# Six digits instead of seven in the threshold search of an expert routing

## What is computed

```python
def _moe_ref(x, w_gate, w1, w2):
    cap = N // E                                   # 2304 // 8 = 288
    order = np.argsort(-(x @ w_gate).flatten())
    for idx in order:                              # best pairs of row and expert first
        tok, e = (int(idx) // E, int(idx) % E)
        if assigned[tok] >= 0 or counts[e] >= cap:
            continue
        assigned[tok] = e; counts[e] += 1
    for e in range(E):
        out[mask] = np.maximum(x[mask] @ w1[e], 0.0) @ w2[e]
def _moe2_ref(x, w_in, w_out, alpha):
    h = x @ w_in
    return (np.maximum(h, 0.0) + alpha * np.minimum(h, 0.0)) @ w_out
```

## Time and profile before

| | us |
|---|---|
| three runs | 1071.69, 1072.57, 1073.44 |
| median | 1072.57 |
| span of the profiled execution | 1067.7 |
| device time of the profiled execution | not listed; its span is 4.9 below the median of the runs |
| PE, DVE, ACT, POOL busy | 926.5, 702.5, 370.7, 357.0 |

### The profile page before, as it was taken

The page is one execution under the profiler, slowest core; times in us unless marked ns, Lnnn a source line. Parts: engine busy times, 40 slices in busy tenths (PEclk is TensorE's granted clock), DMA queues, the critical chain, the costliest instruction groups (busy, mean ns, idle before and its releaser), DMA issues.

```text
span 1067.7 us, 23789 instructions
## 1 busy us (share of the span) xinstructions
PE 926.5 (87%) x8288; PEld 871.3 (82%) x8288; DVE 702.5 (66%) x1860; ACT 370.7 (35%) x1093; POOL 357.0 (33%) x332
## 2 busy tenths in 40 slices
PE   4788898991159999998999899899989999999996
PEld 3677787881148998998899799889979998999995
DVE  6787978758855775675577557656765775675342
ACT  5666676654322114212311321241133124214311
POOL 4463635337545025303601430270144026105401
PEclk9999999995559999999999999999999999999999
DMA  7726363117531212021211202120230212023000
GB/s 156 166 62 148 78 141 79 31 38 196 160 105 44 59 55 71 24 80 47 80 53 54 79 24 80 45 75 23 75 95 24 80 44 68 16 80 102 23 1 22
DMA packets 122571, 76.99 MB, mean 72 GB/s; under 512 B 64328, under 2 KB 105288, under 8 KB 122440
## 3 DMA queue, kind: packets, MB, share of 16 engines
q1 hardware_dynamic: 119368, 65.83, 23.1%
q0 software_dynamic: 3072, 9.44, 3.0%
HBM read 65.81 MB, written 9.44 MB: 70 GB/s over the span
## 4 chain that ended last, share of the span: by engine, by line
PE 58%; DVE 15%; issue 12%; ACT 7%; POOL 6%; DMA 1%; SPq 0%; DVEq 0%; POOLq 0%; ACTq 0%
PE bank L927 15%; PE bank L929 14%; PE bank L928 14%; ACT prob L573 3%; POOL w1s L1414 3%; PE bank L937 3%; DVE onehot L1143 3%; PE bank L390 2%; POOL turning L1422 2%; DVE place L1141 2%; ACT kT L565 2%; PE bank L326 2%; DVE place L1142 2%; DVE nbias L483 1%; PE bank L405 1%
## 5 line engine op out<-in xcount | busy, mean ns | idle before, releaser
L1382 ACT CAST hid<-act 128x288 fp32r<-128x288 f32 x128 | 55.4, 433 | 361.7 <-DVE act L1239 361.7
L927 PE MATMUL bank<-hid,wout 128*128 128x288 f32 x512 | 155.9, 304 | 5.4 <-DVE hid L1245 5.4
L927 PE MATMUL bank<-xy,win 128*128 128x288 f32 x512 | 155.2, 303 | 2.3 <-DVE xy L1230 2.3
L929 PE MATMUL bank<-hid,wout 128*128 128x288 f32 x512 | 152.5, 298 | 0.0
L928 PE MATMUL bank<-hid,wout 128*128 128x288 f32 x512 | 151.3, 296 | 0.0
L928 PE MATMUL bank<-xy,win 128*128 128x288 f32 x512 | 151.3, 295 | 0.0
L929 PE MATMUL bank<-xy,win 128*128 128x288 f32 x512 | 150.8, 294 | 0.0
L1422 POOL DMA_INDIRECT turning<-x_rows,id_new x24 | 24.2, 1007 | 349.6 <-DVE id_new L1213 344.7
L1237 DVE TENSOR_SCALAR neg<-bank,alph 128x288 f32<-128x288 f32 x128 | 66.2, 517 | 101.0 <-PE bank L929 98.9
L1414 POOL TENSOR_TENSOR w1s<-raw,w1s 128x512 fp32r<-128x512 f32 x64 | 86.5, 1353 | 115.7 <-ACT w1s L1351 115.5
L573 ACT ACTIVATE prob<-bank,nbias 96x102 f32<-96x102 f32 (+1 forms) x256 | 86.7, 346 | 50.2 <-DVE nbias L483 34.2
(11 more groups left out here) (184 smaller groups left out, 2254.2 us busy)
## 6 DMA issues: line engine op xcount, KB each, us to landing
raw<-in_moe_w SPq DMA_DIRECT2D x128, 256.0 KB, 3.4
qn<-in_q SPq DMA_DIRECT2D x48, 96.0 KB, 2.3
kn<-in_k SPq DMA_DIRECT2D x48, 96.0 KB, 2.4
vn<-in_v SPq DMA_DIRECT2D x4, 1152.0 KB
x_rows<-xs SPq DMA_DIRECT2D x24, 192.0 KB, 2.1
raw<-in_moe_w_in SPq DMA_DIRECT2D x16, 256.0 KB, 4.0
raw<-in_moe_w_out SPq DMA_DIRECT2D x16, 256.0 KB, 3.7
vw<-in_v SPq DMA_DIRECT2D x16, 204.0 KB
```

The source lines that it names most:

```text
L927: nc.tensor.matmul(out_ap, a_hi, b_hi, start=start, stop=False)
L929: return nc.tensor.matmul(out_ap, a_hi, b_lo, start=False, stop=stop)
L1382: nc.scalar.copy(hid[:, (FC + j) % 3, 0, :], act[:, j % 2, :]).then_inc(h_hi, 1)
```

## The change

The key is read as digits of 5, 5, 5, 5, 6 and 6 bits. There are six levels; levels 4 and 5 compare with 64 values instead of 32 (1536 elements on DVE, products of 64 columns on PE). The digits get their radix added by two instructions instead of one. `PIECES` falls from 18 to 16. The eight low halves that DVE makes in the first routing stood at pieces 2, 4, ... 16; now they stand at 2, 4, ... 14 and 15.

```diff
+DIGIT_BITS = [5, 5, 5, 5, 6, 6]
...
-    BITS = J.bit_length() - 1
-    SHIFTS = list(range((32 - 1) // BITS * BITS, -1, -BITS))
-    LEVELS = len(SHIFTS)
+    LEVELS = len(DIGIT_BITS)
+    SHIFTS = [sum(DIGIT_BITS[l + 1:]) for l in range(LEVELS)]
+    RADIX = [1 << bits for bits in DIGIT_BITS]
...
-    at_least = onehot[:].rearrange("p t m -> p (t m)")[:, 0:NT * J].rearrange("p (t j) -> p t j", t=NT)
+    flat_onehot = onehot[:].rearrange("p t m -> p (t m)")
+    at_least = [flat_onehot[:, 0:NT * j].rearrange("p (t j) -> p t j", t=NT) for j in RADIX]
...
+            radix = RADIX[i // 2]
             if i % 2 == 0:
                 for t in range(NT):
-                    last = nc.tensor.matmul(pR[0:E, 0:J], choice[:, t, :], at_least[:, t, :],
+                    last = nc.tensor.matmul(pR[0:E, 0:radix], choice[:, t, :], at_least[i // 2][:, t, :],
                                             start=(t == 0), stop=(t == NT - 1))
             else:
-                last = nc.tensor.matmul(pR[0:T, 0:J], f["ones"][0:E, :], enough[:], start=True, stop=True)
+                last = nc.tensor.matmul(pR[0:T, 0:radix], f["ones"][0:E, :], enough[:, 0:radix], start=True, stop=True)
...
             do(v.tensor_copy(digits[:], digits_i[:]))
-            do(v.tensor_scalar(digits[:, 1:, :], digits[:, 1:, :], float(J), None, ALU.add), wait=False)
+            for l in range(1, LEVELS):
+                if RADIX[l] != RADIX[l - 1] or l == 1:
+                    same = [m for m in range(l, LEVELS) if set(RADIX[l:m + 1]) == {RADIX[l]}]
+                    do(v.tensor_scalar(digits[:, l:same[-1] + 1, :], digits[:, l:same[-1] + 1, :], float(RADIX[l]), None,
+                                       ALU.add), wait=False)
...
-                    do(v.tensor_scalar(any_v[:], pR[0:T, 0:J], 0.0, None, ALU.is_gt, ALU.add, accum_out=reach[:]))
-                    do(v.tensor_scalar(here, place[:, (l - 1) % 2, :], reach[:], float(J), ALU.subtract, ALU.mult))
+                    do(v.tensor_scalar(any_v[:, 0:above], pR[0:T, 0:above], 0.0, None, ALU.is_gt, ALU.add, accum_out=reach[:]))
+                    do(v.tensor_scalar(here, place[:, (l - 1) % 2, :], reach[:], float(radix), ALU.subtract, ALU.mult))
...
-    DVE_UNIT = {2 * m + 2: m for m in range(DVE_RES)}
+    DVE_UNIT = {min(2 * m + 2, PIECES - 1): m for m in range(DVE_RES)}
```

More of the change, by code:

```diff
@@ L799, in experts @@
     J = f["digit_at"].shape[1]
-    BITS = J.bit_length() - 1
-    SHIFTS = list(range((32 - 1) // BITS * BITS, -1, -BITS))
-    LEVELS = len(SHIFTS)
+    LEVELS = len(DIGIT_BITS)
+    SHIFTS = [sum(DIGIT_BITS[l + 1:]) for l in range(LEVELS)]
+    RADIX = [1 << bits for bits in DIGIT_BITS]
+    assert sum(DIGIT_BITS) == 32 and max(RADIX) == J
     RAW = 8
@@ L1079, in experts @@
     n_steps = [0]
-    STEPS = 9 + LEVELS + 3 + 3 * (LEVELS - 1) + 4 + 7 + 5 + 4 + 3 + 7 + 5 + 3 + 2
+    STEPS = 9 + LEVELS + 2 + len(set(RADIX[1:])) + 3 * (LEVELS - 1) + 4 + 7 + 5 + 4 + 3 + 7 + 5 + 3 + 2
     def stepper(e, k):
@@ L1116, in dve_prepare @@
             for l, shift in enumerate(SHIFTS):
-                do(v.tensor_scalar(digits_i[:, l, :], key[:], shift, J - 1, ALU.logical_shift_right, ALU.bitwise_and),
+                do(v.tensor_scalar(digits_i[:, l, :], key[:], shift, RADIX[l] - 1, ALU.logical_shift_right, ALU.bitwise_and),
                    wait=l == LEVELS - 1)
@@ L1135, in dve_route @@
             l = i // 2
+            radix, above = RADIX[l], RADIX[l - 1]
             here = place[:, l % 2, :]
@@ L1138, in dve_route @@
                 if l > 0:
-                    do(v.tensor_scalar(any_v[:], pR[0:T, 0:J], 0.0, None, ALU.is_gt, ALU.add, accum_out=reach[:]))
-                    do(v.tensor_scalar(here, place[:, (l - 1) % 2, :], reach[:], float(J), ALU.subtract, ALU.mult))
+                    do(v.tensor_scalar(any_v[:, 0:above], pR[0:T, 0:above], 0.0, None, ALU.is_gt, ALU.add, accum_out=reach[:]))
+                    do(v.tensor_scalar(here, place[:, (l - 1) % 2, :], reach[:], float(radix), ALU.subtract, ALU.mult))
                     do(v.tensor_tensor(here, here, digits[:, l, :], ALU.add))
-                ask(v.tensor_tensor(at_least, bc(here, 2, [T, NT, J]), bc(f["digit_at"][:], 1, [T, NT, J]), ALU.is_ge))
+                each = [T, NT, radix]
+                ask(v.tensor_tensor(at_least[l], bc(here, 2, each), bc(f["digit_at"][:, 0:radix], 1, each), ALU.is_ge))
             else:
-                ask(v.tensor_scalar(enough[:], pR[0:E, 0:J], cap8[:], None, ALU.is_ge))
+                ask(v.tensor_scalar(enough[:, 0:radix], pR[0:E, 0:radix], cap8[:], None, ALU.is_ge))
         elif i == 2 * LEVELS:
-            do(v.tensor_scalar(any_v[:], pR[0:T, 0:J], 0.0, None, ALU.is_gt, ALU.add, accum_out=reach[:]))
+            above = RADIX[LEVELS - 1]
+            do(v.tensor_scalar(any_v[:, 0:above], pR[0:T, 0:above], 0.0, None, ALU.is_gt, ALU.add, accum_out=reach[:]))
             here = place[:, (LEVELS - 1) % 2, :]
@@ L1502, in attention_then_experts @@
     E = w_gate.shape[1]
-    T, J = 96, 32
+    T, J = 96, 1 << max(DIGIT_BITS)
     NT = B * S // T
@@ L1520, in attention_then_experts @@
         fixed = route_consts(nc, lasting, T, NT, E, J)
-        early = early_buffers(lasting, T, NT, E, J, LEVELS=7, JT=NT // E, RAW=8, DM=H * D, FC2=w_in.shape[1] // 128)
+        early = early_buffers(lasting, T, NT, E, J, LEVELS=len(DIGIT_BITS), JT=NT // E, RAW=8, DM=H * D, FC2=w_in.shape[1] // 128)
         psum = [whole.enter_context(nc.psum_tensor(f"bank{i}", [128, 512], F32)) for i in range(8)]
```

## The result

The changed kernel takes **1056.36 us** (median of 4 runs, 1050.43 to 1056.88) against 1072.13 for the kernel before in the same session: a ratio of 0.9834, with a 95% interval of 0.9806 to 0.9863. So it is faster by about 16 us; the forecast was 6.5 (1066.1), and its range ended at 1061.5. The profiled execution took 1056.76 us with a span of 1055.0. It lies near its median, and the one before lies low: the spans differ by 12.7 us and the medians by 15.8, so the traces can account for 12.7 only.

A forecast was written before the change was run, and what follows sets the result against it. PE was taken to bound the looped passes, DVE and POOL the first routing. Passes -5.3 and first routing -1.2 made -6.5 us off the median 1072.57: 1066.1 us, range 1061.5 to 1070.8.

The forecast's parts named there:

- one level less: Looped passes: PE loses one level of small products with the gaps at its edges, -1.1 us a pass, -7.7 in all.
- 64 columns on PE, two levels: Looped passes: 24 products of 64 columns cost PE 0.05 us more a level, +0.7 over fourteen levels.
- level 4 waits for DVE: Looped passes: DVE's wider comparison uses up 0.58 us of slack, so PE waits 0.2 a pass, +1.5 in all.
- level 5 delays `xy`: Looped passes: no slack, so 0.80 us of wider comparison delays the low half the first `third` needs, +5.6 in all.
- the tail wait: End of a pass: PE's 0.78 us wait for unit 14's low half goes as the preparation moves earlier, -5.4 in all.
- The first routing: Head before the looped passes: -3.5 for a level, +1.6 comparisons, +0.6 PE columns, +0.1 additions, together -1.2 us.
- the low half that leaves level 6: First routing: 1.7 us of level 6's 6.33; it moves to a later piece, so not counted as saved.
- the collisions of level 6: First routing: POOL operations that collided with level 6 hit what follows, so 3.5 us saved was taken instead of 4.6.
- 2, "more is won": No wait at level 4, whole contended level gained in the first routing, two fewer collisions: -11.1, 1061.5 us; chance 0.13.
- 1: End of a pass: the wait moves one step earlier instead of going, -1.1 in all, 1071.5 us; chance 0.14.
- 3: Looped passes: one more POOL operation ahead of DVE, 1.27 us a pass, +2.4 in all, 1075.0 us; chance 0.06.
- 4: PE's products of 64 columns cost their columns in full, 0.34 us: +4.0, 1070.1 us; chance 0.07.

The follow-up runs named there:

- the kernel whose `xy` waits for PE: The changed kernel with digits of 5, 5, 6, 5, 5, 6 bits and piece 9 given two places instead of one; 1072.58 us.
- the fastest kernel: The changed kernel with digits 5, 5, 6, 5, 5, 6, pieces 9 and 0 two places long, first running-sum part two places instead of three; 1043.65 us.

## Why the prediction was wrong, point by point

**The failed step: what bounds the kernel.** The prediction took a looped pass to be PE at work "with short waits", and its sum compares two passes by the pieces and their order alone. It thereby costed the jump back at the same in both. The page had "issue" at 12% of the chain, and 9.0 us of PE's idle time released by "issue" in five waits; I gave them no price and did not ask whether the change, which moves every instruction behind it in PE's stream, moves them too. What the runs showed in its place is that the changed kernel loads none of its loop again (34 packets instead of 79), and that idle instructions alone do the same for the kernel before (1073.9 to 1059.7). The two kernels run at both kinds of place give its size: 14 to 15 us by the medians, 10.9 and 14.2 by the passes of the profiled executions. For the kernel before, 9.0 of it are the waits themselves. They bring others, 0.35, 0.46 and 1.18 in the rows behind a pass's start, so that a jump back makes 4.0 of waits there, against 1.67 without it. The passes agree: 95.35 against 92.70 where both ends of a pass are jumps back. The 3 us between the 10.9 of the passes and the 14 of the medians are not explained.

**The passes by themselves**, the moved kernel before against the changed one, clean passes of 92.70 and 91.71:

| term, us a pass | forecast | measured |
|---|---|---|
| one level less | -1.1 | -1.37 (the rest of the difference) |
| 64 columns on PE, two levels | +0.1 | +0.24 |
| level 4 waits for DVE | +0.21 | +0.21 |
| level 5 delays `xy` | +0.8 | +0.87 |
| the tail wait | -0.77 | -0.94 |
| sum | -0.76 | -0.99 |

The seven passes sum to 652.82 and 647.49, with their stretches at the lower clock: -5.3. That this is the forecast to the digit is luck, since the changed kernel has one stretch more, which costs 1.45; by the clean passes it is -6.9. The `xy` and tail entries are spacings between starts (0.60 to 1.47, and 1.07 to 0.13), which hold a little more than the idle time.

- *One level less.* I took away the time of three units from the time to the tie piece. What that missed is that each piece slows the starts around it: the product ahead of it is 0.22 to 0.24 before it instead of 0.13, and the second product behind it has 0.24. Around the two pieces of a level this makes 0.88 + 0.34 = 1.22 us over the wide products' own time. The last 0.15 of the -1.37 stays open.
- *Wide products.* 24 starts of 64 columns are (0.86 - 0.193) / 23 = 29.0 ns apart, the last product alone taking 0.193. The Trainium skill, "TensorE: Matmul & The Clock Gate", section "Wait — 56ns, not 53.3ns?", gives 2.5 ns beside the columns' own time, an estimated 29.2 for 64, and the trace agrees with it. I had taken 0.05 us for 24 products, and they take 0.11, with 0.01 more for the second piece of the level.
- *Level 4.* Right in size. The comparison met POOL in this pass (2.65 us instead of 1.75, 806.26 to 808.91), as the one of 1.94 us did in the rows before, and PE starts 0.05 behind its end.
- *Level 5* and *the tail* were right, and each has its own experiment: 8.3 to 2.7 where no wide level stands ahead of `xy`, and 0 to 9.8 where the preparation goes back.

**The first routing** was forecast at -1.2 and gave -0.2 (69.97 against 70.19). The moved kernel before had 70.72, and the three moved changed ones had 69.96 to 70.31, so a difference of this size is within scatter. Up to the end of the last level it gained 3.5 us: `any_v` is read at 283.13, 38.86 behind the logits, against 42.36 before. By the prediction's terms that would be 2.9, the 1.2 and the 1.7 of the low half that leaves level 6. Then 3.3 was given back. Rows after, of a wide comparison that met POOL and of what stands behind the levels:

```profile
271.27 2.77 DVE L1153 TENSOR_TENSOR onehot<-place,digit_at 96x1536 bf16<-96x1536 f32 x1
272.39 4.45 POOL L1425 TENSOR_TENSOR win<-raw,win 128x512 fp32r<-128x512 f32 x2
...
274.09 1.44 PE L941 MATMUL bank<-onehot,choice 96*8 96x64 bf16 x24 [4.77 <-DVE onehot L1153]
...
286.95 1.30 POOL L1425 TENSOR_TENSOR win<-raw,win 128x512 fp32r<-128x512 f32 x1 [2.05 <-ACT win L1362]
...
287.15 1.12 DVE L1168 TENSOR_TENSOR full<-taken,need 96x8 f32<-96x8 f32 x1
...
288.31 1.21 DVE L1169 TENSOR_TENSOR full<-full,first_wins 96x8 f32<-96x8 f32 x1
...
289.74 1.00 DVE L1171 TENSOR_SCALAR sel<-full,fullest 96x8 f32<-96x8 f32 x1
...
304.94 1.12 POOL L1433 DMA_INDIRECT turning<-x_rows,id_new  x1 [14.23 <-DVE id_new L1224]
```

Three operations of 8 elements take 1.0 to 1.2 us instead of 0.16 to 0.23, each until an operation of POOL ends: 2.8 us. The low half of DVE that left level 6 stands here as well, 0.69. POOL had the same 24 low halves to make. Before, it was through with them at 284.9, 44.2 us behind the logits; now DVE was 3.5 us further along, and POOL, which had waited 2.05 for ACT, was through 46.5 behind them. The prediction said that the collisions of level 6 would meet what follows, and took 1.1 of the level's 4.6 off for it; they cost 2.8. The term that was mis-sized is this one. The gather starts 60.67 us behind the logits, before 60.86.

Of the rivals, 2, "more is won", has the number nearest to the result (1061.5) but not its mechanism: the wait at level 4 stayed, and the first routing kept nothing. That its number is nearest is luck. 1, 3 and 4 did not happen. The case that did, instructions loaded again, is none of the four.

## What to carry to other kernels

A loop that is jumped back to has a place in the instruction stream as well as a length. Look at the packets of the instruction queue and at waits for "issue" at a loop's start before pricing anything else, and repeat a surprising gain with the old kernel moved by idle instructions: it may be had without the change. Where two engines get in each other's way, a piece taken from one of them may only move the collisions: here 3.5 us won up to the end of the levels became 0.2, with the other engine's work unchanged. And a wide operation belongs behind what the bound engine asks for next, not ahead of it.

## What the runs showed of the hardware

- **Instruction loading.** In these kernels a loop of PE over eight blocks of 256 instructions is loaded again, with 9 packets of 16 KB, in every pass that follows a jump back; one over seven is not loaded again at all (the six places in the table above). PE stands still for 1.6 to 2.0 us each time in the kernel before and 2.5 to 3.2 in the moved changed kernel. The Trainium skill, "Runtime: NRT & Kernel Launch", section "Instruction fetch mechanics", gives PE room for 2048 instructions, which are eight blocks; it would fit that seven are kept with one being loaded ahead, but no run here shows that, and why eight are not kept stays open. The same section speaks of a window of two blocks for jumps back, and the seven blocks kept here speak against that for PE.
- **The clock falls behind a short wait.** PE's wait of 1.67 us for the first comparison is followed by about 3 us at a granted clock of 0.50 (1.2 GHz) in some of passes 1 to 6 and not in others: in 2 in the changed kernel, 1 and 3 in the same kernel moved by 256 and by 60, 1 in the moved kernel before, 4 with the preparation put back, 5 in each of the two kernels with no wide level ahead of `xy`, and 1 in the kernel whose `xy` waits for PE, where it follows four of the waits of 2.9 us instead. Each costs 1.45 us in the changed kernel. In the fastest kernel, where the wait is 0.94, none of the six has it. What decides it stays open.
- **A wait that no view lists.** PE's 0.21 at level 4 appears only as a wider spacing of starts, 0.44 instead of 0.23.
